# Attention, FFN and mixture of experts in one kernel: the second part of expert 0 counted up to the capacity, its early rows kept in tiles of their own, and four blocks of expert weights split behind the FFN instead of two

## The reference

```python
def _moe2_ref(x, w_gate, w1, w2, capacity):
    ...
    cap = N // E * 2                       # in the setup: 1536 // 8 * 2 = 384
    ...
    for i in range(N):
        e = expert_idx[i]
        if counts[e] < capacity:
            disp[e, counts[e]] = x[i]
            ...
    h = np.maximum(np.einsum('ecd,edf->ecf', disp, w1), 0.0)
    y = np.einsum('ecf,efd->ecd', h, w2)
    ...
        if keep[i]:
            out[i] = gate_w[i] * y[expert_idx[i], pos[i]]
```

## Time and profile before

| | us |
|---|---|
| median of 3 runs (442.56 to 444.22) | 443.85 |
| the profiled execution's own time | 443.4 |
| its span, first to last instruction | 441.7 |
| TensorE busy | 416.1 (94%) |
| VectorE busy | 258.0 (58%) |
| GpSimd busy | 228.5 (52%) |
| ScalarE busy | 198.1 (45%) |

### The profile page before, as it was taken

The page is one execution under the profiler, slowest core; times in us unless marked ns, Lnnn a source line. Parts: engine busy times, 40 slices in busy tenths (PEclk is TensorE's granted clock), DMA queues, the critical chain, the costliest instruction groups (busy, mean ns, idle before and its releaser), DMA issues.

```text
span 441.7 us, 9365 instructions
## 1 busy us (share of the span) xinstructions
PE 416.1 (94%) x3270; PEld 399.1 (90%) x3270; DVE 258.0 (58%) x533; ACT 198.1 (45%) x454; POOL 228.5 (52%) x239
## 2 busy tenths in 40 slices
PE   6799999999999999999999999999699999999892
PEld 5688889999999999999999998899699999998672
DVE  6888866766435333454347665827085775825950
ACT  2789943341311113111233333436638687536840
POOL 3999716454323533144355671504917495527952
PEclk9999999999999999999999999999979999999998
DMA  7996034536970100000003361186664776807400
GB/s 250 398 358 199 3 114 134 165 91 215 355 282 1 54 1 0 0 18 36 0 1 106 97 207 38 44 274 243 180 198 135 244 217 213 284 26 227 160 29 10
DMA packets 34339, 61.89 MB, mean 140 GB/s; under 512 B 4798, under 2 KB 27310, under 8 KB 34288
## 3 DMA queue, kind: packets, MB, share of 16 engines
q1 hardware_dynamic: 31280, 55.92, 39.0%
q0 software_dynamic: 3008, 5.29, 3.5%
HBM read 47.92 MB, written 15.18 MB: 143 GB/s over the span
## 4 chain that ended last, share of the span: by engine, by line
PE 50%; PEld 19%; issue 8%; DVE 7%; POOL 6%; ACT 5%; DMA 3%; PEldq 0%; POOLq 0%; ACTq 0%; DVEq 0%
PE bank L1353 20%; PE bank L1368 20%; PEld bank L1545 9%; PEld bank L1583 8%; POOL w_low L626 3%; ACT scores L672 3%; DMA out<-y_out,token 2%; PE bank L1483 2%; PE bank L1474 2%; PE bank L1320 1%; DVE scores L950 1%; PEld bank L1607 1%; PEld bank L1512 1%; PE bank L1284 1%; ACT w_high L655 1%
## 5 line engine op out<-in xcount | busy, mean ns | idle before, releaser
L549 POOL TENSOR_TENSOR g_low<-act_full,g_high 128x384 fp32r<-128x384 f32 x63 | 63.7, 1011 | 114.8 <-ACT g_high L701 114.8
L701 ACT ACTIVATE g_high<-act_full 128x384 fp32r<-128x384 f32 x64 | 33.7, 526 | 150.1 <-DVE act_full L1014 137.5
L1353 PE MATMUL bank<-x_split,w_high 128*128 (+1 forms) x384 | 98.4, 337 | 0.0
L1008 DVE TENSOR_SCALAR neg<-bank,alpha_sb 128x384 f32<-128x384 f32 x64 | 39.3, 613 | 70.9 <-PE bank L1353 70.8
L626 POOL TENSOR_TENSOR w_low<-w_raw,w_high 128x384 fp32r<-128x384 f32 x48 | 50.0, 1072 | 43.1 <-ACT w_high L793 43.1
L1353 PEld LDWEIGHTS bank<-x_split,w_high 128*128 128x128 f32 x384 | 69.1, 188 | 0.2 <-issue 0.2
L1368 PE MATMUL bank<-w_high,g_high 128*128 128x384 f32 x189 | 65.3, 345 | 0.6 <-POOL g_low L549 0.6
L1353 PE MATMUL bank<-x_split,w_low 128*128 (+1 forms) x192 | 64.5, 336 | 0.0
L1368 PE MATMUL bank<-w_high,g_low 128*128 128x384 f32 x189 | 63.8, 338 | 0.0
L1368 PE MATMUL bank<-w_low,g_high 128*128 128x384 f32 x189 | 63.8, 338 | 0.0
L927 DVE TENSOR_TENSOR w_low<-w_raw,w_high 128x384 fp32r<-128x384 f32 x44 | 32.1, 732 | 22.9 <-ACT w_high L655 22.8
(11 more groups left out here) (164 smaller groups left out, 858.7 us busy)
## 6 DMA issues: line engine op xcount, KB each, us to landing
w_raw<-chunks SPq DMA_DIRECT2D x96, 192.0 KB, 3.7
w_raw<-chunks SPq DMA_DIRECT2D x32, 384.0 KB, 3.4
rk_in<-att_rk SPq DMA_DIRECT2D x12, 704.0 KB, 6.3
routed_rows<-fill SPq DMA_DIRECT2D x1, 5211.0 KB, 17.7
xe<-routed_rows SPq DMA_DIRECT2D x7, 579.0 KB, 4.3
v_in<-att_v SPq DMA_DIRECT2D x12, 200.0 KB, 6.0
out<-fill SPq DMA_DIRECT2D x1, 2304.0 KB, 23.9
x_split<-x_split POOLq DMA_DIRECT2D x18, 48.0 KB, 2.6
```

Source lines behind the costliest of these rows:

```text
L549: pool.tensor_tensor(gl[:, f % 4, :], act_full[:, f % 2, :], gh[:, f % 4, :].bitcast(f32), ALU.subtract).then_inc(s_gl, 1)
L701: act.activation(gh[:, f % 4, :], act_full[:, f % 2, :], ACT.Copy).then_inc(s_gh, 1)
L1008: dve.tensor_scalar(neg[:, f % 2, :], h, 0.0, alpha_sb[:, f:f + 1], ALU.min, ALU.mult)\
L1353: last = mm(bank[f % 4][:, 0:G], a[:, f, w], x[:, kc, bass.ds(g * G, G)], start=kc == 0 and i == 0, stop=kc == KC - 1 and i == 2)
```

## The change

1. `counts` of expert 0 becomes `min(CNT, CAP)` minus the early part, with `CAP` = 384.
2. The early rows get tiles of their own, `early_token` and `early_gate`; `keep_meta(1)` no longer waits for `s_outa`, and `early_scatter` stands ahead of the last four splits on GpSimd. (`y_copy(1)` still waits for `s_outa`.)
3. `DEFER` goes from 2 to 4: the last FFN group splits blocks 16 to 23, blocks 24 to 27 are split with `early_relu` 4 to 7, and blocks 28 to 31 in expert 0. There, in the two-tile form, they follow blocks 3 to 6; in the one-tile form they stand at the end, where three of them stood near the start. SyncE loads all four behind the tokens of expert 1.
4. In the early part TensorE's order is finer: `early_up(0)` and `early_up(1)` are cut in two around `turn_rows` and `logits`, `turn_logits` comes ahead of `early_up(2)`, `positions` ahead of `early_up(3)`; VectorE does `choose` ahead of `early_low(1)`.

```diff
-    DEFER = 2
+    DEFER = 4
...
+    early_token = mlp.take("early_token", [P, ET], i32)
+    early_gate = mlp.take("early_gate", [P, ET], f32)
...
             sp.dma_start(xe[:, 1, 0:ET, :], disp[0:ER, :].rearrange("(i p) n -> p i n", p=P)).then_inc(s_xea, 16)
-            for m in range(DEFER):
-                load_chunk(2 * NF - RAW + m, m)
...
             load_xe(1)
-            for m in range(DEFER, RAW):
+            for m in range(RAW):
                 load_chunk(2 * NF - RAW + m, m)
...
-            for c in range(2 * NF - 4 - DEFER, 2 * NF):
-                split_low(c)
             def early_scatter(i):
...
-                    out=out, out_offset=bass.IndirectOffsetOnAxis(ap=token[:, 1, i:i + 1], axis=0),
+                    out=out, out_offset=bass.IndirectOffsetOnAxis(ap=early_token[:, i:i + 1], axis=0),
...
+            for c in range(2 * NF - 4 - DEFER, 2 * NF - 4):
+                split_low(c)
+            for i in reversed(range(ET)):
+                early_scatter(i)
+            for c in range(2 * NF - 4, 2 * NF):
+                split_low(c)
...
-                if e == 0:
-                    for i in reversed(range(ET)):
-                        early_scatter(i)
...
-            for f in range(3):
+            for f in range(2):
                 early_relu(f)
             gate_exp(NG - 1)
-            early_relu(3)
+            for f in range(2, 4):
+                early_relu(f)
             for f in range(4, 4 + DEFER):
                 split_high(2 * NF - 8 - DEFER + f)
                 early_relu(f)
-            early_relu(6)
-            split_high(2 * NF - 4)
-            early_relu(7)
...
                     if e == 0:
                         xe_high(0, 2, bank[6])
-                        for c in range(2 * NF - 3, 2 * NF):
-                            split_high(c)
...
                     act.sem_inc(s_fc[1], 2)
+                    if e == 0:
+                        for c in range(2 * NF - 4, 2 * NF):
+                            split_high(c)
...
             early_low(0)
             logits_copy(NG - 1)
+            choose(NG - 1)
             early_low(1)
-            choose(NG - 1)
             places(NG - 1)
...
                 dve.wait_ge(s_gone, max(e - 1, 0) + C_GONE)
-                if e == 1:
-                    dve.wait_ge(s_outa, 16 * ET)
...
-            dve.tensor_tensor(counts[0:1, 0:1], CNT[:, 0:1], base_0[0:1, :], ALU.add).then_inc(s_cnti, 1)
+            dve.scalar_tensor_tensor(counts[0:1, 0:1], CNT[:, 0:1], float(CAP), base_0[0:1, :], ALU.min, ALU.add)\
+               .then_inc(s_cnti, 1)
...
                     low2(3, 4, 5, 6, 7)
+                    if e == 0:
+                        for c in range(2 * NF - 4, 2 * NF):
+                            split_low(c)
...
-            early_up(0)
-            turn_rows(q)
-            early_up(1)
+            early_up(0, (0, 1))
+            turn_rows(q, (0, 1))
+            early_up(0, (2,))
+            turn_rows(q, (2,))
+            early_up(1, (0, 1))
             logits(q)
+            early_up(1, (2,))
+            turn_logits(q)
             early_up(2)
-            turn_logits(q)
+            positions(q)
             early_up(3)
-            positions(q)
             early_up(4)
```

More of the change, by code:

```diff
@@ L763, in early_y @@
                 act.activation(y_out[:, 1, i, :], bank[4 + i][:, 0:DM], ACT.Copy,
-                               scale=gate[:, 1, i:i + 1]).then_inc(s_ayo, 1)
-            for f in range(3):
+                               scale=early_gate[:, i:i + 1]).then_inc(s_ayo, 1)
+            for f in range(2):
                 early_relu(f)
             gate_exp(NG - 1)
-            early_relu(3)
+            for f in range(2, 4):
+                early_relu(f)
             for f in range(4, 4 + DEFER):
@@ L772, in _ @@
                 early_relu(f)
-            early_relu(6)
-            split_high(2 * NF - 4)
-            early_relu(7)
-            assert NFE == 8 and DEFER == 2
+            assert NFE == 4 + DEFER
             def relu(e, f, n):
@@ L868, in _ @@
                             xe_high(0, 2, bank[6])
-                        if e == 0 and 3 <= f < 6:
-                            split_high(2 * NF - 6 + f)
+                        if e == 0 and 3 <= f < 7:
+                            split_high(2 * NF - 7 + f)
                         if f in TURN and e < E - 1:
@@ L1166, in _ @@
             early_low(6)
+            split_low(2 * NF - 2 - DEFER)
             dve.wait_ge(s_xea, 16)
-            dve.tensor_copy(token[:, 1, 0:ET], xe[:, 1, 0:ET, DM:DM + 1].rearrange("p a b -> p (a b)"))
-            dve.tensor_copy(gate[:, 1, 0:ET], xe[:, 1, 0:ET, DM + 1:ROW].rearrange("p a b -> p (a b)"))\
+            dve.tensor_copy(early_token[:, :], xe[:, 1, 0:ET, DM:DM + 1].rearrange("p a b -> p (a b)"))
+            dve.tensor_copy(early_gate[:, :], xe[:, 1, 0:ET, DM + 1:ROW].rearrange("p a b -> p (a b)"))\
                .then_inc(s_metaa, 1)
             early_low(7)
-            split_low(2 * NF - 4)
+            split_low(2 * NF - 1 - DEFER)
             dve.wait_ge(s_cnti, 2)
@@ L1232, in _ @@
                             keep_meta(0)
-                        if e == 0 and 3 <= f < 6:
-                            split_low(2 * NF - 6 + f)
+                        if e == 0 and 3 <= f < 7:
+                            split_low(2 * NF - 7 + f)
                         if f in TURN and e < E - 1:
@@ L1370, in products, with turn_rows @@
                 return last
-            def turn_rows(q):
-                for i in range(GT):
+            def turn_rows(q, tiles=range(GT)):
+                for i in tiles:
                     pe.wait_ge(s_x2, q * GT + i + 1)
@@ L1461, in _, with early_up @@
                 last.then_inc(s_tile if i < GT - 1 else s_step, 1)
-            def early_up(f):
+            def early_up(f, kcs=range(KC)):
                 pe.wait_ge(s_wl1, NF + f + 1)
@@ L1470, in early_up @@
                     pe.wait_ge(s_agl, f - 3)
-                for kc in range(KC):
+                for kc in kcs:
                     w = slice(kc * P, (kc + 1) * P)
@@ L1475, in early_up @@
                                   start=kc == 0 and i == 0, stop=kc == KC - 1 and i == 2)
-                last.then_inc(s_ah, 1)
+                if kcs[-1] == KC - 1:
+                    last.then_inc(s_ah, 1)
             def early_down(i, f):
```

## The result

The changed kernel took 435.86 us (median of 4 runs, 435.51 to 436.83), the kernel before 443.72 on the same chip: 0.983 of it, 95% interval 0.9805 to 0.9855. So it is faster, by 7.9 us. The time lies in the range on record, but the likeliest time was 431.2, a gain of 12.45: over a third of it is missing. The profiled execution took 436.0 us, with a span of 434.3. The forms of the work came out as forecast: the page's row of two-tile passes counts 96, where the earlier trace rows had 120.

What follows compares the result with a forecast made beforehand. The prediction took TensorE, busy 94% of the span, to bound the kernel. Its terms, 7.4 + 7.55 + 1.0 - 3.5 = 12.45 us gained, led to a forecast of 431.2 us, range 428.3 to 436.2.

Steps and rivals of the forecast that it cites:

- part 1: Expert 0: the capped count makes one tile of two, 10.95 us instead of 18.33, gain 7.4 us.
- rival B: Expert 1: VectorE is shut out through a GpSimd run, loss about 8.5 us, time 436.1 us; chance 0.15.
- Part 2: Expert 1: the 5.3 us wait and 2.25 us from half clock go, gain 7.55 us.
- The late blocks: Expert 1: four block splits moved into expert 0 delay `relu_low` and the next tokens' low part, loss 3.5 us.
- Rival A: Expert 1: the four late block splits cost almost nothing, 0.9 to 1.2 us, time 428.6 us; chance 0.2.
- The early stretch: Early part and last FFN group: waits for `g_low` (0.6 us) and `carried` (0.3 us) go, gain 1.0 us.
- The sum: Whole kernel: gains of 7.4, 7.55 and 1.0 less a loss of 3.5 give 12.45 us.

Runs made afterwards that it cites:

- e10: The kernel before with TensorE's experts written without branches, only the bodies that run for these tokens; 442.9 us, ratio 0.9985.
- e5: The changed kernel with TensorE's experts written without branches, only the bodies that run for these tokens; 431.3 us, ratio 0.9726.
- e4: The changed kernel with the old count, so expert 0 keeps its two tiles; 437.0 us, ratio 0.9817.
- e11: As e5, but GpSimd leaves out the low part of W1 of expert 2; 428.9 us, ratio 0.9676.
- e8: The changed kernel with expert 2's loads held back as in e1 and VectorE's two small early copies moved ahead of `early_low(5)`; 433.3 us, ratio 0.9761.
- e1: The changed kernel with SyncE holding expert 2's loads until TensorE has done the first step of expert 0's down part; 433.6 us, ratio 0.9758.
- e2: The changed kernel with the two bodies that expert 0 doesn't run (406 instructions) left out of TensorE's program; 440.0 us, ratio 0.9904.
- e6: As e5, without branches in TensorE's experts, but with the old count, so expert 0 has two tiles; 436.0 us, ratio 0.9826.

## Why the prediction was right in part, and where it failed

**The step that failed is part 1's price.** It took off "the 1.00 us wait that is shown ahead of expert 6, whose cause is the W1 split of a later expert and which expert 0 hasn't". The work of expert 0 was priced well: 11.01 us without branches, for 10.95. The wait was misread. It goes when the jumps go (e10), and by the packets it is the fetch of instructions behind the body that a one-tile expert jumps past; expert 0 has it worse. Its second part starts amid the full loads, where the packet comes 3 us late, so that it pauses in the middle (1.93 us) and once more at its end (2.94); 0.4 more go around them. The gain was 2.0 us instead of 7.4. That the time still lies in the range, 0.3 us inside its upper end, is luck: that end was priced by rival B, whose cause did not come about, and these pauses were on no list.

GpSimd's timeline of the kernel before would have warned: the last W1 splits that expert 6 needs had ended at 403.13, 7 us ahead of the wait that was put down to them.

```profile
401.13 2.00 POOL L626 TENSOR_TENSOR w_low<-w_raw,w_high 128x384 fp32r<-128x384 f32 x2 [0.33 <-ACT w_high L793]
```

The Trainium skill, "Runtime: NRT & Kernel Launch", section "Instruction fetch mechanics", says that instructions come in blocks of 16 KiB ahead of their use, and that a taken branch whose target isn't at hand stalls until its block is fetched. The runs agree, with 2.4 to 3.5 us from the packet to TensorE's next pass. They add two things. Beside the loads a packet came 3.0 us later (301.75 against 298.75). And the number of blocks is that of the whole program, whichever bodies run: 31 of 32 with the old count and the new, 21 of 22 in e5.

**Part 2, the waits of expert 1, was right.** e4, in which no branch of experts 0 and 1 goes another way than before, shows 18.00 us for expert 1 (forecast 17.91).

**The late blocks: right in mechanism, hidden in the result.** In the changed kernel no wait for `relu_low` or the low part is seen, as TensorE itself is late; half clock costs the 2.5 us instead. Where TensorE is on time, expert 1 takes 20.88 us for a forecast of 21.4, with the two waits named: 0.75 for `relu_low` (forecast 0.9) and 1.34 for the next tokens' low part. e11 parts them: 1.7 us are VectorE shut out by GpSimd's run, 1.3 are ScalarE late. Rival A was wrong (the late blocks cost 3.0 us in e5), and so was rival B, though its 436.1 is the nearest number: the clock did fall again, which was the sign given for it, but not for VectorE.

**The early stretch** gave 0.5 for 1.0. Both waits went; the copy that was caught took 0.5 back.

**The sum.** Without branches on TensorE it stands at 11.6 for 12.45. With them the profiles show 7.5 up to expert 2's first pass: 12.45, less 5.4 in part 1, less 0.5 in the early stretch, and 0.9 more in expert 1 than forecast. From there to the end both kernels take the same, within 0.1.

What stays open: why the pause ahead of expert 1 grows by about as much as an earlier start or a prompt first packet gives (2.94, 3.79, 4.28 and 4.62 us, but 2.76 in e8). In all five it ends 2.8 to 3.5 us behind its packet, so the open point is when that packet falls. Not every jump costs something either: the changed kernel goes from expert 1 to expert 2 past the body of the third tile, a packet falls at 326.0, and expert 2 starts at 329.24 without a pause. Open is also whether a layout of the code keeps all bodies and has no pause; none of these runs shows one. The fastest kernels that leave out no work are e5, for these tokens only (431.3), and, with every branch kept, e8 and e1 (433.3 and 433.6, not told apart).

## What to carry to other kernels

When a change makes an engine jump past more code, price the jump: look for gaps that the profile puts down to "issue" or to a releaser long done, and for a packet of the instruction queue some 3 us ahead of their end. A price taken from a neighbour (here expert 5's) has to be taken with all its waits, unless the releaser's own times show the cause of each. A pause on the engine that bounds the kernel also hides what would be late next, so taking it away gives less than its length.

## What was not expected of the hardware

- Behind a taken branch TensorE stood still until 2.4 to 3.5 us after a packet of 16 KB of instructions, also with the DMA engines nearly idle (408.75 to 411.87 in e2). In the experts without branches such packets caused no pause, also beside full loads (303.0 in e5, 300.25 in e6).
- Leaving out 406 instructions that are never run made the kernel some 3 us slower (0.9904 of the kernel before instead of 0.983), by pauses of 2.98, 3.08 and 1.78 us some 100 us later, and by half clock behind two of them.
- A copy of 128x2 on VectorE took 4.20 us beside four GpSimd splits and 0.15 us when it stood two splits earlier, ahead of them; VectorE's splits of 128x384 in expert 1 took 1.01 us beside GpSimd's run in e5 and 0.56 without it in e11.
